# Two places for the parts of an expert tile's tokens, and a new order around the first two expert tiles

## The chip, the cores and the metric

The kernel runs on one core of one Trainium2 chip. The metric is the device time of one execution in microseconds (us); the median of three runs is given, and one further execution was profiled. A core has TensorE (PE; its weight loads are PEld), VectorE (DVE), ScalarE (ACT), GpSimd (POOL) and SyncE (SP, which here only issues DMAs). Each engine works through its own list of instructions in order, and they meet at semaphores alone: `then_inc` raises one when an instruction has finished, `wait_ge` holds its engine until it has a value.

## The reference

Three layers over 2304 tokens of width 512, all in float32:

```python
scores = q @ k.T / 8                          # 4 batches x 8 heads, 576 tokens, 64 wide
attn = softmax(scores where >= the 32nd largest of the row)
x = attn @ v                                  # 2304 x 512
x = softplus(x @ w_in) @ w_out                # 512 -> 2048 -> 512
logits = x @ w_gate                           # 8 experts
e = argmax(logits);  gate = softmax(logits)[e]
out = gate * (relu(x @ w1[e]) @ w2[e])        # 512 -> 1024 -> 512, the token's own expert
```

## The kernel before

Matmuls run at a fast rate that rounds its operands, so each operand is split in two parts, hi (the rounded value) and lo (what is left), and `product` adds three matmuls: hi by hi, hi by lo, lo by hi. ScalarE makes the hi part, VectorE or GpSimd the lo part.

**Attention and the dense layer** take the first three quarters. The 2304 tokens are 18 pieces of 128, and two pieces make a group of the dense layer. For each group `up` and `down` run over 8 units of w_in and w_out, with the attention of later groups between them. `down(g, u, part)` (L648) is half of a unit's down-projection, six matmuls of 512 columns; the last group's units are called by `last_down(u)`, which does both halves.

**Routing.** A piece that is done is turned (`turn_tokens`, L667) and its 8 logits are computed by `logits` (L678), four matmuls of 8 columns. From the logits VectorE makes the choice of expert (`choose`) and the gate (`gates`). TensorE counts how many tokens before each one went to the same expert: `count_early` for the first 16 pieces, `count_late` (L705) for the last two. From the counts VectorE works out for every token its tile of 128 and its lane in the tile, then TensorE makes tables of the tiles from them (`slots_early`, and `slots_late`, L712, 18 matmuls). `in_slots`, `slot_values` and `lane_hots` on VectorE make the operands of slots_late. The first two expert tiles belong to the expert with most tokens among the first 16 pieces and are filled from these, so their tables are there early.

**An expert tile T.** GpSimd gathers its 128 tokens into `xs` (an indirect DMA). TensorE turns them with `turn_xs(T, place)` (L722), four instructions into bank 0 of PSUM. ScalarE copies that out as `xsT_hi` (`xs_out`, L1013) and VectorE forms `xsT_lo` (`xs_low`, L1340). `e_up(T)` (L741) is 8 products, two halves (n) of 512 columns with four steps (kk) each, into banks 1 and 2. Their rectification is half on ScalarE (`e_relu_out`, L1020) and half on VectorE (`relu`, L1333); both raise `e_relu`. `turn_h(T)` (L764) turns the 1024 hidden values, 8 instructions into banks 3 and 4, `e_h_out` and `h_low` split them, and `e_down(T)` (L774) is 8 products. `y_out` scales by the gate and GpSimd scatters the rows. With one place for xsT_hi and xsT_lo, the tokens of the next tile can be copied out only when e_up of the tile before is done (`act.wait_ge(e_h_raw, T)`).

**The order** is written out by hand for each engine. `amid` names calls that are made ahead of a product inside another call: in `e_up` by (n, kk), in `e_down` by kk. Around the end of the dense layer TensorE does, in this order: turn_xs(0), last_down(6), the first half of e_up(0), last_down(7), the second half of e_up(0) with the turns and logits of the last two pieces in it, turn_xs(1), turn_h(0), e_up(1) with count_late after its first product, e_down(0) with turn_h(1) and slots_late at its products 4 and 5, e_down(1). VectorE does in this stretch: the lo parts of the first expert's weights (`first_w1`, `first_w2`), relu(0), choose, xs_low(1), gates, the chain from the counts to `abs_tile`, h_low(0), in_slots, slot_values, lane_hots, relu(1), and after slots_late the tables, h_low(1) and y_out(0). For the later tiles all engines run the same loop: on TensorE turn_h(T), e_up(T+1), turn_xs(T+2), e_down(T).

The SBUF space behind xsT_lo was an unused gap of the size of both parts.

Of the kernel before, what the change touches and what calls it, by code (L numbers as in the profile page):

```python
# [20 lines left out]
def build(nc, q, k, v, w_in, w_out, w_gate, w1, w2, out):  # L21
# [97 lines left out]
    with ExitStack() as ctx:  # L119
        def sb(name, shape, dt=F32):  # L120
            return ctx.enter_context(nc.sbuf_tensor(name, shape, dt))
# [87 lines left out]

        wbuf = sb("wbuf", [P, 3, WLEN])  # L210
        sb("gap_d", [P, WLEN])
        xsT_hi = sb("xsT_hi", [P, KD, P], F32R)
        xsT_lo = sb("xsT_lo", [P, KD, P], F32R)
        sb("gap_x", [P, 2 * KD * P])
        xs = sb("xs", [P, XS, DM])
        inslot = sb("inslot", [P, NT, 4, NTAB], F32R)
        hr = sb("hr", [P, EF])
# [329 lines left out]
        def _(pe):  # L547
# [121 lines left out]
            def turn_tokens(g, kk, bank):  # L669
                nonlocal turns  # L670
                pe.wait_ge(y_copied, kk + 1)
                if bank == 5:
                    pe.wait_ge(h_copied, UNITS * (g + 1))
                turns = kk + 1
                for m in range(KD):
                    mm = nc.tensor.transpose(psum[:, bank, m * P:(m + 1) * P],
                                             x2tok[:, kk % 2, m * P:(m + 1) * P], ident[:])
                mm.then_inc(turned, 1)  # L678

            def logits(kk, bank):  # L680
                nonlocal logit_turns
                if kk == 0:
                    pe.wait_ge(wg_loaded, 16)
                pe.wait_ge(turn_copied, kk + 1)
                for m in range(KD):
                    mm = nc.tensor.matmul(psum[:, bank, 0:E], x2T[:, kk % 2, m, :], wg[:, m, :],
                                          start=(m == 0), stop=(m == KD - 1))
                mm.then_inc(logits_raw, 1)
                logit_turns = kk + 1
# [31 lines left out]
            def turn_xs(T, place):  # L721
                pe.wait_ge(gathered[place], T // XS * 16 + 16)  # L722
                if not (isinstance(T, int) and T == 0):
                    pe.wait_ge(xs_split, T)
                for kk in range(KD):
                    mm = nc.tensor.transpose(psum[:, 0, kk * P:(kk + 1) * P],
                                             xs[:, place, kk * P:(kk + 1) * P], ident[:])
                mm.then_inc(xs_turned, 1)
# [4 lines left out]
            def product(ps, x_hi, x_lo, par, at, start, stop):  # L733

                hi = w_hi[:, par * 2, at:at + 512]
                lo = wbuf[:, par * 2, at:at + 512].bitcast(F32R)
                nc.tensor.matmul(ps, x_hi, hi, start=start, stop=False)  # L737
                nc.tensor.matmul(ps, x_hi, lo, start=False, stop=False)  # L738
                return nc.tensor.matmul(ps, x_lo, hi, start=False, stop=stop)  # L739

            def e_up(T, rank=None, amid=(), halves=False, parts=(0, 1)):  # L741
                rank = rank_at(T) if rank is None else rank
                if halves and 0 in parts:
                    pe.wait_ge(quarter_split, 2)
                elif not halves:
                    pe.wait_ge(w1_split, rank + 1)
                if 0 in parts:
                    pe.wait_ge(xs_split, T + 1)
                    if not (isinstance(T, int) and T == 0):
                        pe.wait_ge(e_relu, T * 2)  # L750
                par = rank % 2
                for n in parts:
                    if n and halves:
                        pe.wait_ge(quarter_split, 3)
                        pe.wait_ge(w1_split, 1)
                    for kk in range(KD):
                        if (n, kk) in amid:
                            amid[n, kk]()
                        mm = product(psum[:, 1 + n, :], xsT_hi[:, kk, :], xsT_lo[:, kk, :], par,
                                     kk * EF + n * 512, kk == 0, kk == KD - 1)  # L760
                if 1 in parts:
                    mm.then_inc(e_h_raw, 1)
# [60 lines left out]
            def last_down(u):  # L823
                for part in range(2):
                    down(LASTG, u, part)

            up(LASTG, 0)
            for part in range(2):
# [20 lines left out]
            rank_first = rank_at(0)  # L849
            turn_xs(0, 0)  # L850
            last_down(6)
            e_up(0, rank_first, halves=True, parts=(0,))
            last_down(7)
            e_up(0, rank_first, {(1, 1): lambda: turn_tokens(LASTG, NT - 2, 5),
                                 (1, 2): lambda: turn_tokens(LASTG, NT - 1, 4),
                                 (1, 3): lambda: logits(NT - 2, 3)}, halves=True, parts=(1,))
            logits(NT - 1, 7)
            turn_xs(1, 1)
            turn_h(0)
            e_up(1, rank_first, {(0, 1): count_late})  # L860
            e_down(0, 0, rank_first, {KE // 2: lambda: turn_h(1), KE // 2 + 1: slots_late}, halves=True)
            e_down(1, 1, rank_first, {KE - 2: lambda: turn_xs(2, 2)})
            pe.wait_ge(tiles_ready, 1)
            e_up(2)
            turn_xs(3, 3)
            _, live = live_below(pe)

            def tile(T, place, live):
                turn_h(T)
                with live(T + 1):  # L870
                    e_up(T + 1)
                with live(T + 2):
                    turn_xs(T + 2, (place + 2) % XS)
                e_down(T, place % 2)
# [5 lines left out]
        def _(act):  # L880
# [98 lines left out]
            def logits_out(kk, bank):  # L979
                act.wait_ge(logits_raw, kk + 1)  # L980
                nc.scalar.copy(lg[:, kk, :], psum[:, bank, 0:E]).then_inc(logits_copied, 1)
# [28 lines left out]
                act.wait_ge(w2_loaded[0] if n else w2_first, 32)  # L1010
                nc.scalar.copy(w_hi[:, 0, at], wbuf[:, 0, at]).then_inc(w2_hi if n else first_hi, 1)

            def xs_out(T):  # L1013
                act.wait_ge(xs_turned, T + 1)
                if not (isinstance(T, int) and T == 0):
                    act.wait_ge(e_h_raw, T)
                nc.scalar.copy(xsT_hi[:].rearrange("p k t -> p (k t)"),
                               psum[:, 0, :]).then_inc(xs_copied, 1)

            def e_relu_out(T):  # L1020
# [91 lines left out]
                first_w1((u - 3) // 2, (u - 3) % 2)  # L1112
            rectify(LASTG, 7)
            logarithm(LASTG, 7)
            xs_out(0)
            h_high(LASTG, 7)
            first_w2(0)
            first_w2(1)
            down_out(LASTG)
            turn_out(NT - 2, 5)  # L1120
            turn_out(NT - 1, 4)
            logits_out(NT - 2, 3)
            logits_out(NT - 1, 7)

            e_relu_out(0)
            xs_out(1)
            gate_exps(1)
            e_h_out(0, 0)
            e_relu_out(1)
            e_h_out(1, 1)  # L1130
            xs_out(2)
            act.wait_ge(splits_ready, 1)
            early_split(act, 1, split_w1)
            next_expert(act, 1, split_w2)
# [2 lines left out]
            def tile(T, place, live):  # L1137
                e_relu_out(T)
                with live(T + 1):
                    xs_out(T + 1)  # L1140
                e_h_out(T, place % 2)
                early_split(act, T, split_w1)
                with live(T + 1):
                    next_expert(act, T, split_w2)
# [4 lines left out]
        def _(dve):  # L1149
# [187 lines left out]
                nc.vector.tensor_scalar(hr[:, 512:EF], psum[:, 2, :], 0.0, None,  # L1337
                                        ALU.max).then_inc(e_relu, 1)

            def xs_low(T):  # L1340
                dve.wait_ge(xs_copied, T + 1)
                nc.vector.tensor_tensor(xsT_lo[:].rearrange("p k t -> p (k t)"), psum[:, 0, :],
                                        xsT_hi[:].rearrange("p k t -> p (k t)").bitcast(F32),
                                        ALU.subtract).then_inc(xs_split, 1)

            def h_low(T, hpar):
# [34 lines left out]

            for q in range(4):
                first_w1(q // 2, q % 2)
            xs_low(0)
            first_w2(0)
            first_w2(1)

            relu(0)
            dve.wait_ge(logits_copied, NT)
            choose(LAST, 1)  # L1390
            xs_low(1)
            gates(LAST, 1)
            dve.wait_ge(counts_ready, 2)
            then(nc.vector.tensor_copy(new_count[:].rearrange("p t e -> p (t e)"),
# [13 lines left out]
            then(nc.vector.tensor_reduce(abs_tile[:], pos3[:], AX.X, ALU.add))  # L1408
            then(nc.vector.tensor_tensor(abs_tile[:], abs_tile[:], reltile[:], ALU.add))
            h_low(0, 0)  # L1410
            in_slots(inslot, abs_tile, slice(0, NT), NTAB)
            slot_values(inslot, slice(0, NT), NTAB)
            lane_hots(LAST).then_inc(lanes_ready, 1)
            relu(1)

            then(nc.vector.tensor_tensor(prod[:], perm[:], bc(need[:], EE, 1), ALU.mult))
            then(nc.vector.tensor_reduce(ntile[:], prod[:], AX.X, ALU.add))
# [34 lines left out]
                then(nc.vector.tensor_tensor(prod[:], match[:], bc(values, EE, 1), ALU.mult))  # L1452
                then(nc.vector.tensor_reduce(by_rank[:, i, :], prod[:], AX.X, ALU.add))
            nc.vector.tensor_copy(by_rank_i[:], by_rank[:]).then_inc(ranks_ready, 1)
            xs_low(2)
            y_out(1, 1)


# [16 lines left out]
            early_split(dve, 1, split_w1)  # L1475
            next_expert(dve, 1, split_w2)
            relu(2)
            xs_low(3)
            _, live = live_below(dve)

            def tile(T, place, live):
                h_low(T, place % 2)
                early_split(dve, T, split_w1)
                with live(T + 1):
                    next_expert(dve, T, split_w2)
                    relu(T + 1)
                with live(T + 2):
                    xs_low(T + 2)
                y_out(T, place)

            later_tiles(dve, tile, live)
# [203 lines left out]
```

## Time and profile before

| | us |
|---|---|
| median of three runs | 1056.23 (1055.35 to 1056.42) |
| profiled execution | 1057.04 |
| its span, first to last instruction | 1054.8 |
| TensorE busy in the span | 992.9 |
| VectorE busy | 817.3 |
| ScalarE busy | 727.6 |
| GpSimd busy | 711.9 |

The span is what the trace shows; the execution's own time is 2.2 us longer. Times in a timeline count from the start of the span. A row gives start, duration, engine, line, operation, output<-inputs and the number of like instructions merged into it; in brackets stands the engine's idle time before it and what ended it. Matmuls overlap: the distance from one start to the next is what one costs, not its duration. The granted clock of TensorE (PEclk) is a share of 2.4 GHz; it has two levels here, 1.00 and 0.50, and its mean over the span is 0.983.

### The profile page before, as it was taken

The numbers are of one execution on the slowest core, as the hardware profiler recorded it, in microseconds if no ns is written. First come the engines' busy times: TensorE is split into PE (matmuls) and PEld (weight loads), VectorE is DVE, ScalarE is ACT, GpSimd is POOL, SyncE is SP. The second block draws the span as 40 slices with busy tenths as digits, with TensorE's granted clock in tenths as the row PEclk, the third lists the DMA queues.
The fourth block names the chain that finished last, engine by engine and source line by source line (L and its number), as shares of the span: only waits on it lengthen the run. The fifth ranks groups of instructions, "written<-read, shape, count | busy, mean of one in ns | idle before, by whom it ended". The sixth has DMA issues, their size and how long they took to land.

```text
span 1054.8 us, 21596 instructions
## 1 busy us (share of the span) xinstructions
PE 992.9 (94%) x6878; PEld 806.3 (76%) x6879; DVE 817.3 (77%) x1744; ACT 727.6 (69%) x1390; POOL 711.9 (67%) x831
## 2 busy tenths in 40 slices
PE   5565899999999999999999999999999999999996
PEld 2343687788788788788788888887887788888875
DVE  7999999999999999999999999994345622222261
ACT  3888898988998998998888999998554111111140
POOL 2688898889899899899888899899351311111101
PEclk9996899999999999999999999999999999999999
DMA  9723253343344343324434333333481421111100
GB/s 311 257 91 127 112 171 121 128 143 121 114 153 165 114 157 121 124 98 144 169 119 155 117 120 102 121 121 121 156 331 54 165 96 52 40 40 40 40 20 20
DMA packets 43391, 130.99 MB, mean 124 GB/s; under 512 B 4320, under 2 KB 18656, under 8 KB 33056
## 3 DMA queue, kind: packets, MB, share of 16 engines
q1 hardware_dynamic: 40256, 120.09, 32.5%
q0 software_dynamic: 3040, 9.70, 2.7%
q8 instruction: 51, 0.84, 0.3%
q14 instruction: 44, 0.36, 0.1%
HBM read 111.95 MB, written 18.09 MB: 123 GB/s over the span
## 4 chain that ended last, share of the span: by engine, by line
PE 80%; DVE 8%; POOL 4%; ACT 3%; issue 3%; DMA 1%; SPq 1%; ACTq 0%; DVEq 0%; POOLq 0%
PE psum L614 8%; PE psum L575 7%; PE psum L644 7%; PE psum L737 6%; PE psum L739 6%; PE psum L738 6%; PE psum L646 6%; PE psum L645 6%; PE psum L663 6%; PE psum L665 6%; PE psum L664 6%; PE psum L589 5%; DVE top L1158 3%; DVE work L1164 3%; PE psum L769 2%
## 5 line engine op out<-in xcount | busy, mean ns | idle before, releaser
L1158 DVE MAX8 top<-work 128x8 f32<-128x576 f32 x432 | 305.4, 752 | 0.0
L1164 DVE MATCH_REPLACE8 work<-top,work 128x576 f32<-128x576 f32 x288 | 212.6, 749 | 0.0
L644 PE MATMUL psum<-x_parts,wi_hi 128*128 128x256 f32 x576 | 171.1, 297 | 0.0
L645 PE MATMUL psum<-x_parts,wi_hi 128*128 128x256 f32 x576 | 162.9, 283 | 0.0
L646 PE MATMUL psum<-x_parts,wi_lo 128*128 128x256 f32 x576 | 162.7, 283 | 0.0
L614 PE MATMUL psum<-prT,vtok 128*64 128x128 f32 (+3 forms) x1600 | 117.1, 287 | 15.2 <-ACT prT L918 15.2
L614 PEld LDWEIGHTS psum<-prT,vtok 128*64 128x64 f32 (+1 forms) x1600 | 85.5, 144 | 54.2 <-issue 41.2
L575 PE MATMUL psum<-kT,qT 64*128 64x512 f32 (+3 forms) x640 | 113.0, 480 | 11.5 <-DMA qT<-in_q 4.4
L1638 POOL DMA_INDIRECT out<-ys,dst_now x19 | 19.2, 1012 | 152.6 <-DVE ys L1360 150.7
L663 PE MATMUL psum<-wo_ring,h_hi 128*128 x288 | 119.1, 414 | 1.0 <-POOL h_lo L1547 0.9
L1541 POOL TENSOR_TENSOR hs<-hs,ab 128x512 f32<-128x512 f32 x72 | 93.7, 1301 | 32.7 <-ACT ab L941 32.5
L644 PEld LDWEIGHTS psum<-x_parts,wi_hi 128*128 128x128 f32 x576 | 109.9, 191 | 6.8 <-issue 2.4
L905 ACT ACTIVATE pr<-pr,bias 128x576 f32<-128x576 f32 x144 | 110.0, 766 | 6.7 <-POOL pr L1536 3.7
L665 PE MATMUL psum<-wo_ring,h_lo 128*128 x288 | 113.1, 393 | 0.0
L664 PE MATMUL psum<-wo_ring,h_hi 128*128 x288 | 112.7, 391 | 0.0
L645 PEld LDWEIGHTS psum<-x_parts,wi_hi 128*128 128x128 f32 x576 | 110.1, 191 | 0.2
L646 PEld LDWEIGHTS psum<-x_parts,wi_lo 128*128 128x128 f32 x576 | 110.1, 191 | 0.0
L911 ACT ACTIVATE pr<-pr,rden 128x576 f32<-128x576 f32 x144 | 104.4, 784 | 8.0 <-DVE rden L1175 8.0
L575 PEld LDWEIGHTS psum<-kT,qT 64*128 64x128 f32 (+1 forms) x640 | 57.5, 195 | 68.1 <-issue 59.4
L589 PE MATMUL psum<-ident,pr 128*128 128x128 f32 x576 | 81.3, 284 | 22.3 <-ACT sc L890 16.7
L1547 POOL TENSOR_TENSOR h_lo<-hs,h_hi 128x512 fp32r<-128x512 f32 x72 | 93.1, 1293 | 5.9 <-ACT h_hi L949 5.9
L589 PEld LDWEIGHTS psum<-ident,pr 128*128 128x128 f32 x576 | 66.6, 145 | 27.9 <-issue 17.6
(215 smaller groups left out, 2353.1 us busy)
## 6 DMA issues: line engine op xcount, KB each, us to landing
wo_ring<-wo_parts SPq DMA_DIRECT2D x72, 1024.0 KB, 4.8
wo_parts<-wo_ring SPq DMA_DIRECT2D x8, 1024.0 KB, 3.8
kT<-in_k SPq DMA_DIRECT2D x16, 288.0 KB, 3.4
qT<-in_q SPq DMA_DIRECT2D x16, 288.0 KB, 3.9
vtok<-in_v SPq DMA_DIRECT2D x16, 256.0 KB, 2.9
wo_raw<-in_moe_w_out SPq DMA_DIRECT2D x1, 4096.0 KB, 14.1
wi_raw<-in_moe_w_in SPq DMA_DIRECT2D x4, 1024.0 KB, 14.4
x_rows<-x2tok SPq DMA_DIRECT2D x16, 256.0 KB, 2.4
```

The source lines that it names most:

```text
L575: mm = nc.tensor.matmul(to[rows, :], qT[h * HD:(h + 1) * HD, p, cols], kT[h * HD:(h + 1) * HD, p, keys], start=True, stop=True)
L589: mm = nc.tensor.transpose(transit[:, j // 3, j % 3 * P:(j % 3 + 1) * P], pr_of(n)[:, first_key(t) + c * P:first_key(t) + (c + 1) * P], id ...
L614: mm = nc.tensor.matmul(x_raw_at[h * HD:(h + 1) * HD, cols], vtok[rows, p, c, h * HD:(h + 1) * HD], probs, start=(c == 0), stop=(c == FULL))
L644: nc.tensor.matmul(ps[:, part, :], wi_hi[:, u, kk, f], hi, start=first, stop=False)
L645: nc.tensor.matmul(ps[:, part, :], wi_hi[:, u, kk, f], lo, start=False, stop=False)
L646: mm = nc.tensor.matmul(ps[:, part, :], wi_lo[:, u, kk, f], hi, start=False, stop=last)
L663: nc.tensor.matmul(psum[:, 6 + a, :], high, hi, start=(f == 0), stop=False)
L664: nc.tensor.matmul(psum[:, 6 + a, :], high, lo, start=False, stop=False)
L665: mm = nc.tensor.matmul(psum[:, 6 + a, :], low, hi, start=False, stop=(f == KF - 1))
L905: nc.scalar.activation(pr[:, n % 2 * 2 + t, :], pr[:, n % 2 * 2 + t, :], ACT.Exp, bias=bias[:, n % 2, 0, t:t + 1], scale=1.0, accum_out=ep ...
L1158: nc.vector.max(top[:, at, 8 * r:8 * r + 8], sc_of(n)[:, t, :] if r == 0 else work[:, t, :]).then_inc(topk_step, 1)
L1164: nc.vector.match_replace(work[:, t, :], top[:, at, 8 * r - 8:8 * r], sc_of(n)[:, t, :] if r == 1 else work[:, t, :], TAKEN).then_inc(topk ...
```

## The change

The two parts get a second place, chosen by the tile's number, odd or even; e_up, xs_out and xs_low take it as an argument, and xs_out now waits for e_up of two tiles before. On TensorE turn_xs(1) moves between the two halves of the last down-projection. E_up(1) no longer stands behind turn_h(0): turn_h(0) is now inside it, ahead of (0, 3), and count_late ahead of (1, 1). In e_down(0), turn_h(1) moves from product 4 to 5 and slots_late from 5 to 6. ScalarE does xs_out(1) before it copies out the last down-projection, and e_relu_out(0) before the last logits. VectorE does xs_low(1) before relu(0), and relu(1) between h_low(0) and in_slots.

```diff
-        xsT_hi = sb("xsT_hi", [P, KD, P], F32R)
-        xsT_lo = sb("xsT_lo", [P, KD, P], F32R)
-        sb("gap_x", [P, 2 * KD * P])
+        xsT_hi = sb("xsT_hi", [P, 2, KD, P], F32R)
+        xsT_lo = sb("xsT_lo", [P, 2, KD, P], F32R)
...
-            def e_up(T, rank=None, amid=(), halves=False, parts=(0, 1)):
+            def e_up(T, xpar, rank=None, amid=(), halves=False, parts=(0, 1)):
...
-                        mm = product(psum[:, 1 + n, :], xsT_hi[:, kk, :], xsT_lo[:, kk, :], par,
+                        mm = product(psum[:, 1 + n, :], xsT_hi[:, xpar, kk, :], xsT_lo[:, xpar, kk, :], par,
...
             turn_xs(0, 0)
             last_down(6)
-            e_up(0, rank_first, halves=True, parts=(0,))
-            last_down(7)
-            e_up(0, rank_first, {(1, 1): lambda: turn_tokens(LASTG, NT - 2, 5),
-                                 (1, 2): lambda: turn_tokens(LASTG, NT - 1, 4),
-                                 (1, 3): lambda: logits(NT - 2, 3)}, halves=True, parts=(1,))
+            e_up(0, 0, rank_first, halves=True, parts=(0,))
+            down(LASTG, UNITS - 1, 0)
+            turn_xs(1, 1)
+            down(LASTG, UNITS - 1, 1)
+            e_up(0, 0, rank_first, {(1, 1): lambda: turn_tokens(LASTG, NT - 2, 5),
+                                    (1, 2): lambda: turn_tokens(LASTG, NT - 1, 4),
+                                    (1, 3): lambda: logits(NT - 2, 3)}, halves=True, parts=(1,))
             logits(NT - 1, 7)
-            turn_xs(1, 1)
-            turn_h(0)
-            e_up(1, rank_first, {(0, 1): count_late})
-            e_down(0, 0, rank_first, {KE // 2: lambda: turn_h(1), KE // 2 + 1: slots_late}, halves=True)
+            e_up(1, 1, rank_first, {(0, 3): lambda: turn_h(0), (1, 1): count_late})
+            e_down(0, 0, rank_first, {KE // 2 + 1: lambda: turn_h(1), KE - 2: slots_late}, halves=True)
             e_down(1, 1, rank_first, {KE - 2: lambda: turn_xs(2, 2)})
             pe.wait_ge(tiles_ready, 1)
-            e_up(2)
+            e_up(2, 0)
             turn_xs(3, 3)
             _, live = live_below(pe)
 
             def tile(T, place, live):
                 turn_h(T)
                 with live(T + 1):
-                    e_up(T + 1)
+                    e_up(T + 1, (place + 1) % 2)
...
-            def xs_out(T):
+            def xs_out(T, xpar):
                 act.wait_ge(xs_turned, T + 1)
-                if not (isinstance(T, int) and T == 0):
-                    act.wait_ge(e_h_raw, T)
-                nc.scalar.copy(xsT_hi[:].rearrange("p k t -> p (k t)"),
+                if not (isinstance(T, int) and T < 2):
+                    act.wait_ge(e_h_raw, T - 1)
+                nc.scalar.copy(xsT_hi[:, xpar].rearrange("p k t -> p (k t)"),
...
             rectify(LASTG, 7)
             logarithm(LASTG, 7)
-            xs_out(0)
+            xs_out(0, 0)
             h_high(LASTG, 7)
             first_w2(0)
             first_w2(1)
+            xs_out(1, 1)
             down_out(LASTG)
             turn_out(NT - 2, 5)
             turn_out(NT - 1, 4)
             logits_out(NT - 2, 3)
+            e_relu_out(0)
             logits_out(NT - 1, 7)
 
-            e_relu_out(0)
-            xs_out(1)
             gate_exps(1)
             e_h_out(0, 0)
             e_relu_out(1)
             e_h_out(1, 1)
-            xs_out(2)
+            xs_out(2, 0)
...
-                    xs_out(T + 1)
+                    xs_out(T + 1, (place + 1) % 2)
...
-            def xs_low(T):
+            def xs_low(T, xpar):
                 dve.wait_ge(xs_copied, T + 1)
-                nc.vector.tensor_tensor(xsT_lo[:].rearrange("p k t -> p (k t)"), psum[:, 0, :],
-                                        xsT_hi[:].rearrange("p k t -> p (k t)").bitcast(F32),
+                nc.vector.tensor_tensor(xsT_lo[:, xpar].rearrange("p k t -> p (k t)"), psum[:, 0, :],
+                                        xsT_hi[:, xpar].rearrange("p k t -> p (k t)").bitcast(F32),
...
-            xs_low(0)
+            xs_low(0, 0)
             first_w2(0)
             first_w2(1)
 
+            xs_low(1, 1)
             relu(0)
             dve.wait_ge(logits_copied, NT)
             choose(LAST, 1)
-            xs_low(1)
             gates(LAST, 1)
...
             h_low(0, 0)
+            relu(1)
             in_slots(inslot, abs_tile, slice(0, NT), NTAB)
             slot_values(inslot, slice(0, NT), NTAB)
             lane_hots(LAST).then_inc(lanes_ready, 1)
-            relu(1)
...
-            xs_low(2)
+            xs_low(2, 0)
...
-            xs_low(3)
+            xs_low(3, 1)
...
-                    xs_low(T + 2)
+                    xs_low(T + 2, place % 2)
```

## Rows read from the trace of the kernel before

**Rows 1.** The page, part 1: busy us, share of span, instructions by engine.
```profile
PE 992.9 (94%) x6878; PEld 806.3 (76%) x6879; DVE 817.3 (77%) x1744; ACT 727.6 (69%) x1390; POOL 711.9 (67%) x831
```

**Rows 2.** Windows, later tiles: us, busy (xcount) PE, PEld, DVE, ACT, POOL, PEclk, DMA, GB/s.
```profile
960.00:1000.00 40.00, 40.00 (x193) 32.99 (x192) 10.27 (x15) 6.44 (x12) 7.24 (x12) 1.00 0.12 39
```

**Rows 3.** Timeline of TensorE: start, duration, instruction, idle before and its releaser.
```profile
806.05 0.95 PE L686 MATMUL psum<-wg,x2T 128*128 128x8 f32 x8
...
807.76 1.91 PE L769 MATMUL psum<-ident,hr 128*128 128x128 f32 x8 [0.27 <-ACT hr L1024]
809.32 0.78 PE L737 MATMUL psum<-w_hi,xsT_hi 128*128 x1
...
810.74 0.44 PE L709 MATMUL psum<-onehot,tri 128*128 128x16 f32 x2
...
816.05 0.39 PE L739 MATMUL psum<-w_hi,xsT_lo 128*128 x1
816.57 0.49 PE L737 MATMUL psum<-w_hi,hrT_hi 128*128 x1
...
820.43 1.07 PE L769 MATMUL psum<-ident,hr 128*128 128x128 f32 x8 [0.80 <-DVE hr L1337]
...
822.04 2.11 PE L716 MATMUL psum<-inslot,lanehot 128*128 128x108 f32 x18
...
826.26 0.47 PE L737 MATMUL psum<-w_hi,hrT_hi 128*128 x1
```

**Rows 4.** Timeline of VectorE, the same stretch.
```profile
798.07 4.50 DVE L1378 TENSOR_TENSOR wbuf<-wbuf,w_hi 128x2048 fp32r<-128x2048 f32 x2 [2.67 <-ACT w_hi L1011]
806.25 0.69 DVE L1337 TENSOR_SCALAR hr<-psum 128x512 f32<-128x512 f32 x1 [3.69 <-PE psum L739]
...
811.62 0.18 DVE L1394 COPY new_count<-psum 128x16 f32<-128x16 f32 x1 [1.77 <-PE psum L710]
...
815.53 1.29 DVE L1350 TENSOR_TENSOR hrT_lo<-psum,hrT_hi 128x512 fp32r<-128x512 f32 x2
...
819.16 0.42 DVE L1260 TENSOR_TENSOR lanehot<-rank,lane 128x256 fp32r<-128x256 f32 x1
819.50 0.68 DVE L1337 TENSOR_SCALAR hr<-psum 128x512 f32<-128x512 f32 x1
...
825.44 1.28 DVE L1350 TENSOR_TENSOR hrT_lo<-psum,hrT_hi 128x512 fp32r<-128x512 f32 x2
```

**Rows 5.** Timelines of ScalarE (ACT), then of GpSimd (POOL).
```profile
801.49 1.08 ACT L970 COPY x2tok<-psum 128x512 f32<-128x512 f32 x2 [1.64 <-PE psum L665]
...
807.10 0.60 ACT L1024 ACTIVATE hr<-psum 128x512 f32<-128x512 f32 x1
...
787.88 0.98 POOL L1625 DMA_INDIRECT xs<-x_rows,src_now  x1 [0.81 <-POOL src_now L1621]
...
824.64 0.18 POOL L1621 COPY src_now<-src_i 128x1 int32<-128x1 int32 x1 [27.03 <-DVE src_i L1431]
```

**Rows 6.** Windows about the clock's fall; PEclk stands before the DMA share.
```profile
804.50:807.80 3.30, 3.04 (x25) 2.67 (x23) 1.18 (x4) 0.98 (x5) 0.00 (x0) 1.00 0.00 0
807.90:811.20 3.30, 3.30 (x14) 3.01 (x14) 1.78 (x9) 1.67 (x4) 0.00 (x0) 0.50 0.02 5
811.30:830.00 18.70, 17.77 (x89) 14.19 (x89) 15.28 (x56) 1.67 (x3) 2.89 (x6) 1.00 0.08 24
```

**Rows 7.** Chain of waits in order of time: start, us, what; full clock.
```profile
756.62 0.49 PE psum L694 x2
757.11 0.22 PE psum L695 x2
...
846.36 0.44 PE psum L726 x4
...
852.18 0.23 PE psum L739
852.41 0.87 PE psum L769 x8
```

## The prediction

> **What bounds the kernel now.** The line of busy time comes first: TensorE works 94% of the span, VectorE 77% [rows 1]. The stages come next, since that share is a mean. While the later expert tiles run (960 to 1000 us) TensorE is busy 40.00 of 40 us, and every instruction that the change touches in the loop over tiles stands there: the places of an expert tile's tokens alternate, but who waits for what, in which order on each engine, stays [rows 2]. Xs_out(T+1) gets a weaker wait on ScalarE, yet e_relu_out(T) ahead of it in the same queue waits for the same matmuls. So the loop can give nothing and lose nothing, and what is won or lost before it arrives at the end in full. That leaves the passage from the last down-projection to the start of e_down(1), 800 to 827 us. There I read the engines one by one: TensorE [rows 3], VectorE [rows 4], ScalarE and GpSimd [rows 5].
>
> What the reader is to see: turn_h(0) starts at 807.76, 0.06 after ScalarE's rectification, which itself stood behind logits_out. Count_late starts at 810.74. From 811.62 VectorE is on one chain: counts, ranks, abs_tile, then h_low(0) at 815.53, and e_down(0) starts at 816.57, when its first half is done. E_up(1) had ended, at 816.3. Then in_slots, lane_hots (ending 819.58), relu(1) (819.50), which turn_h(1) waits for at 820.43 (0.80 idle), slots_late at 822.04, tables, h_low(1) at 825.44, e_down(1) at 826.26. So the passage alternates between TensorE's order and VectorE's chain, and the chain cannot begin before count_late.
>
> **The change, part by part.** Sums are made against the profiled execution: 1057.04 us, span 1054.8, 2.2 outside it. It lies 0.81 above the median of 1056.23.
>
> *Second turn of tokens moved up.* Turn_xs(1) goes ahead of the second half of down(7). It costs TensorE 0.44 warm [rows 7], nothing else: its gather was issued at 787.88, 12 us earlier, and no DMA or GpSimd instruction moves. All behind it up to the end of e_up(0) slides by 0.44: the last matmuls whose end VectorE's relu(0) waits for then end at 806.69 instead of 806.25. On ScalarE xs_out(1) (128x512, the 0.60 of the like rectification; between 801.0 and 801.6) fits into the 1.64 idle ahead of down_out, which wants 801.49 + 0.44 = 801.93. On VectorE xs_low(1), 0.69 as relu, runs at 802.6 behind first_w2, in the 3.69 idle before relu(0). Were that cover gone, down_out and all behind it would be up to 0.6 late. The stores of the last rows go 0.44 later; the gather that needs them waits for the tables until 824.64, 22 us behind. Cost 0, all in the 0.44.
>
> *E_up(1) ahead of turn_h(0).* This is what the second places allow. Relu(0) ends on VectorE at 807.38; ScalarE's, no longer behind logits_out, at 807.3. With 0.2 for the wait (0.06 from ScalarE's relu to turn_h(0), 0.35 from h_low's first half to e_down(0)) e_up(1) starts at 807.6, against 809.32.
>
> *Count_late moved from behind one product to behind five.* A product is three matmuls, 0.23 each [rows 7], 0.70 together before rounding; the first after a pause takes 0.1 more. Nine matmuls: 807.6 + 0.1 + 2.1 = 809.8. Turn_h(0): 0.87 warm [rows 7], 810.66. Two products: 812.06. Count_late 0.45 warm, estimated: 0.63 at the lower clock, and a like four with 128 columns each, where it has 16, took 0.49 + 0.22 [rows 7]. It ends at 812.5. VectorE picks up the counts at 812.65, against 811.62: **1.0 later**. At one clock it would be 2.6 later; in the execution before, TensorE's granted clock was 0.50, its lower level of 1.2 GHz, from 807.9 to 811.3 [rows 6], after sixteen logits matmuls of 8 columns, a turn and a wait of 0.27. Its turn_h took 1.56 instead of 0.87 (807.76 to 809.32), its first product 1.42 instead of 0.70, its count some 0.2 more: 1.6 in all. Now full products stand in that place at once, a turn less stands among the small matmuls and the wait is shorter; I take the clock as staying at 2.4 GHz there. If it falls, those 1.6 come back.
>
> *The xs_low(1) taken out of the chain after choose.* 0.69 off VectorE at 808.3, but VectorE is done with the gates 1.77 before the counts at 811.62; logits_out comes 0.44 later and even so the gates end near 810.1. Worth 0, since count_late is the later.
>
> *H_low(0), then relu(1), then tables.* The chain from counts to h_low(0) is unchanged, 3.91: e_down(0) starts at 816.57 + 1.0 = 817.6. E_up(1) ends at 814.7 (812.5 + nine matmuls), so TensorE waits some 2.8 where it waited 0.3. Relu(1), 0.60, now precedes in_slots: lanes are ready at 819.58 + 1.0 + 0.6 = 821.2.
>
> *Turn_h(1) one product later, slots_late one more.* From 817.6: five products 3.6, turn_h(1) 0.87 with no wait (it saves the 0.80), one product 0.70, so slots_late starts at 822.8, after the lanes. Before: 822.04. **0.75 later.** Its 1.95, the tables and h_low(1) follow as before: the first half of h_low(1), 825.44 + 0.69 before, is there at 826.13 + 0.75 = 826.9. E_down(0) has ended by 826.3, because only two products are left behind slots_late, not three. E_down(1) starts at 827.0 to 827.2, against 826.26: **0.75 to 0.95 later, I take 0.8**. The gather of tile 2, turn_xs(2), xs_low(2) and e_up(2) hang on the same tables and slide alike.
>
> *Second places in SBUF, other addresses in the loop.* No row has a price. From below and above: the later tiles take 40.00 of 40, so there is no idle to take away; a slower read would show in the matmuls' 0.23, of which I see no reason for a change. 0.
>
> Sum: 0 + 0.8 = 0.8 us, 1057.8 in the terms of the profiled execution, **1057.0** against the median.
>
> **The clock, weighed against the Trainium skill.** The row shows the fall at 807.9 and the return by 811.3 [rows 6]; idle alone didn't make it, for 0.80 idle at 819.6 was followed by full clock. The Trainium skill, "TensorE: Matmul & The Clock Gate", Part 1, says that half rate is the default and that activity lifts it, and its Part 4 that turns don't count as busy in the same way. The trace agrees with both as far as it goes. By that rule the 2.8 us of waiting that the change opens is a danger, and the rival below comes out.
>
> **Rivals.**
> 1. *The clock falls in the new wait before e_down(0).* Place: 814.7 to 817.6. The wait is ten times the 0.27 before the fall at 807.76, which speaks for it; against it, full matmuls stand on both sides, and waits of 0.8 passed unharmed. Price: one stretch like that of 807.9 to 811.3, 3.4 at half rate, costs 1.7, on a path that TensorE alone sets up to slots_late. 0.8 + 1.7 = 2.5: 1058.7. With 0.8 lost already it decides once the fall costs 1.3 more, 2.6 us at the lower level.
> 2. *The early fall stays,* inside e_up(1). 1.6 come back: 1058.6. For: logits are still there. Against: the products. Some of the timed executions of before may also have escaped their fall (their spread is 1.07), to the same effect on the difference.
> 3. *TensorE's order decides, not VectorE's chain.* If the counts reached VectorE early enough to hide the chain, TensorE alone would need from 807.6: e_up(1) with turn_h and count 7.1, e_down(0) with turn_h and slots 8.7 with its first matmul: 823.4 instead of 826.26, 2.9 faster: 1053.3. Against it stands the chain of 3.91 + 0.7 behind a count at 812.5. It wants count_late first, and the change puts it last.
>
> **How the numbers follow.** Forecast 0.62, rival 1 0.20, rival 2 0.08, rival 3 0.08, and 0.02 for nothing moved at all. A measurement of this kernel tells about 0.2%, 2.1 us, from no change. The forecast lies within; rivals 1 and 2 mostly beyond (0.23 with their part of the edges), rival 3 is faster. Same 0.68, slower 0.24, faster 0.08. The range runs from 1055.0 (the forecast less an uncertainty of 1.0 in the waits and the 1.0 spread of the runs) to 1059.2 (rivals 1 and 2 with 0.5 on top). The forecast's own range is 1055.8 to 1058.2.
>
> **What would show it.** Right: turn_xs(1) between two halves of down(7) at 0.44; e_up(1) 0.2 after the rectifications; the clock at 1.00 from 804 to 814; the counts' first VectorE instruction 1 us later; an idle of 2.5 to 3 us before e_down(0), released by hrT_lo; no idle before turn_h(1); under 1 us before e_down(1); the later tiles at 40.00 of 40. Wrong: an idle under 1.5 before e_down(0); a clock of 0.50 behind it; the loop's matmuls off 0.23; or a wait for xs_low(1).

## The result, and the profile after

| | us |
|---|---|
| changed kernel, median of nine runs | 1059.37 (1058.29 to 1060.30) |
| kernel before, median of nine runs beside them | 1056.12 (1055.35 to 1058.16) |
| ratio | 1.0030, 95% interval 1.0019 to 1.0040 |
| profiled execution of the changed kernel | 1058.81, span 1056.6 |

Slower by some 3.2 us, where 0.8 was forecast: 1059.37 against a forecast of 1057.0 and a range up to 1059.2. A second timing on another occasion gave a ratio of 1.0028 (1.0017 to 1.0038), 1058.87 against 1056.19.

The profile page's row of busy time and the window over the later tiles, which answer to [rows 1] and [rows 2], read in the changed kernel:

```profile
PE 993.5 (94%) x6878; PEld 806.7 (76%) x6879; DVE 817.3 (77%) x1744; ACT 727.8 (69%) x1390; POOL 711.9 (67%) x831
```

```profile
960.00:1000.00 40.00, 40.00 (x195) 32.99 (x194) 11.66 (x17) 7.52 (x14) 7.24 (x12) 1.00 0.13 40
```

TensorE's work is the same and the loop over the later tiles is as full as before. So the time went in the passage. TensorE there, answering to [rows 3] (start, duration, instruction, in brackets the idle time before it):

```profile
799.47 0.60 PE L725 MATMUL psum<-ident,xs 128*128 128x128 f32 x4
799.83 0.48 PE L662 MATMUL psum<-wo_ring,h_hi 128*128 x1
...
806.06 0.95 PE L685 MATMUL psum<-wg,x2T 128*128 128x8 f32 x8
807.09 0.47 PE L736 MATMUL psum<-w_hi,xsT_hi 128*128 x1
...
809.24 1.04 PE L768 MATMUL psum<-ident,hr 128*128 128x128 f32 x8
...
811.51 0.29 PE L708 MATMUL psum<-onehot,tri 128*128 128x16 f32 x2
...
813.80 0.40 PE L738 MATMUL psum<-w_hi,xsT_lo 128*128 x1
816.98 0.49 PE L736 MATMUL psum<-w_hi,hrT_hi 128*128 x1 [2.78 <-DVE hrT_lo L1349]
...
818.03 0.63 PE L736 MATMUL psum<-w_hi,hrT_hi 128*128 x1
818.45 0.63 PE L737 MATMUL psum<-wbuf,hrT_hi 128*128 x1
...
822.14 1.03 PE L768 MATMUL psum<-ident,hr 128*128 128x128 f32 x8
...
823.71 2.11 PE L715 MATMUL psum<-inslot,lanehot 128*128 128x108 f32 x18
...
827.93 0.47 PE L736 MATMUL psum<-w_hi,hrT_hi 128*128 x1 [0.65 <-DVE hrT_lo L1349]
```

Turn_xs(1) stands at 799.47, between the two halves of down(7), and costs TensorE 0.48 (forecast: 0.44): from the first matmul of down(7) to the first one behind it is 3.19, against 2.71 before. E_up(1) starts at 807.09, right behind the rectifications. The turn before (0, 3) is at full clock and count_late comes at 811.51. Then TensorE stands idle for 2.78 us, released by h_low(0), and behind that wait the matmuls start 0.42 apart, not 0.23. VectorE, answering to [rows 4], shows why e_down(0) waits: the counts are picked up at 812.13 after 2.48 us of idle, and h_low(0) follows 3.91 later, as before; relu(1) follows it at once.

```profile
812.13 0.17 DVE L1393 COPY new_count<-psum 128x16 f32<-128x16 f32 x1 [2.48 <-PE psum L709]
...
816.04 1.29 DVE L1349 TENSOR_TENSOR hrT_lo<-psum,hrT_hi 128x512 fp32r<-128x512 f32 x2
817.24 0.68 DVE L1336 TENSOR_SCALAR hr<-psum 128x512 f32<-128x512 f32 x1
```

The clock of the changed kernel, answering to [rows 6] (the value before the last two):

```profile
807.90:811.20 3.30, 3.30 (x20) 2.82 (x19) 1.23 (x8) 1.29 (x3) 0.00 (x0) 1.00 0.02 5
811.30:816.90 5.60, 2.90 (x15) 2.12 (x13) 4.26 (x19) 0.60 (x1) 0.00 (x0) 1.00 0.00 0
817.50:820.90 3.40, 3.40 (x9) 2.62 (x9) 3.33 (x8) 0.00 (x0) 0.00 (x0) 0.50 0.00 0
```

The fall among the logits is gone, and there is one behind the new wait: 9 matmuls in 3.4 us. ScalarE's copy of the last down-projection, 801.49 in [rows 5], stands at 801.50 here and serves below as the mark from which the passage is measured: over the fourteen profiles of all kernels it lies anywhere from 801.3 to 803.3, and what stands behind the start of e_up(2) took 222.0 to 222.2 in all of them.

```profile
801.50 1.08 ACT L969 COPY x2tok<-psum 128x512 f32<-128x512 f32 x2 [0.81 <-PE psum L664]
```

The first matmul of e_up(2) ends the passage, at 834.44: 32.94 from the mark. In the kernel before it is 832.78, so 31.29. Turn_xs(1) stands ahead of the mark in the changed kernel and behind it before, which adds 0.48 (from the first matmul of down(7) to the mark it is 3.39 against 2.91). These two executions thus differ by 1.65 + 0.48 = 2.13.

### The profile page after: what moved, and what is told of

Same layout as the page of the kernel before. It is cut to its first block, busy times and chain, and to the rows that moved or that the text cites. A ratio compares the mean times of both kernels' runs of the same rounds, so it can differ in the third digit from the quotient of the medians.

```text
span 1056.6 us, 21595 instructions
## 1 busy us (share of the span) xinstructions
PE 993.5 (94%) x6878; PEld 806.7 (76%) x6879; DVE 817.3 (77%) x1744; ACT 727.8 (69%) x1390; POOL 711.9 (67%) x831
## 4 chain that ended last, share of the span: by engine, by line
PE 81%; DVE 7%; POOL 4%; ACT 3%; issue 3%; DMA 1%; SPq 1%; ACTq 0%; DVEq 0%; POOLq 0%
PE psum L613 8%; PE psum L574 7%; PE psum L643 7%; PE psum L736 6%; PE psum L738 6%; PE psum L737 6%; PE psum L645 6%; PE psum L644 6%; PE psum L662 6%; PE psum L664 6%; PE psum L663 6%; PE psum L588 5%; DVE top L1157 3%; DVE work L1163 3%; PE psum L768 2%
```

## Experiments

Each kernel was timed beside the kernel before, and rows with the same value under "before" were timed together. Ratios are to it, with 95% intervals.

| kernel | median | before | ratio |
|---|---|---|---|
| early count | 1055.47 | 1056.66 | 0.9989 (0.9980 to 0.9998) |
| wait filled | 1058.30 | 1056.66 | 1.0018 (1.0009 to 1.0027) |
| relu(1) back | 1058.74 | 1056.66 | 1.0023 (1.0014 to 1.0032) |
| first half of the change | 1056.31 | 1056.66 | 0.9995 (0.9986 to 1.0004) |
| changed kernel again | 1058.87 | 1056.19 | 1.0028 (1.0017 to 1.0038) |
| early count, early slots | 1054.54 | 1056.19 | 0.9984 (0.9974 to 0.9993) |
| count one product earlier | 1058.23 | 1056.32 | 1.0019 (1.0010 to 1.0028) |
| early count and slots, relu(1) back | 1055.78 | 1056.32 | 0.9996 (0.9987 to 1.0005) |

**Early count.**

```diff
-            e_up(1, 1, rank_first, {(0, 3): lambda: turn_h(0), (1, 1): count_late})
+            e_up(1, 1, rank_first, {(0, 2): count_late, (0, 3): lambda: turn_h(0)})
```

> The changed kernel with one thing different: count_late stands ahead of (0, 2) of e_up(1), behind two products, instead of ahead of (1, 1), behind five and turn_h(0). Theory A (VectorE's chain from the counts makes the wait before e_down(0), and the lower clock follows that wait): the counts reach VectorE 3 us earlier, e_down(0) starts without a wait at 814 to 815, the clock reads 1.00 behind it, and the time is 3.5 to 5 us under the changed kernel's, so 1 to 2 under the one before. Theory B (the second places and the other addresses, or the turn inside the down-projection, cost most of the 3.2 us): under 1 us faster than the changed kernel.

It is 1.2 us under the kernel before, where the changed kernel is 2.7 to 3.2 over it: 3.9 to 4.4 between them, as expected. TensorE at e_down(0):

```profile
815.08 0.49 PE L736 MATMUL psum<-w_hi,hrT_hi 128*128 x1 [0.40 <-DVE hrT_lo L1349]
```

The wait is 0.40, not quite the none that was expected, and no fall shows in the passage. VectorE in this kernel says what bounds the counts now:

```profile
810.03 0.16 DVE L1243 TENSOR_TENSOR gate_parts<-gate,gate_parts 128x2 fp32r<-128x2 f32 x1
810.23 0.17 DVE L1393 COPY new_count<-psum 128x16 f32<-128x16 f32 x1
```

The last gate instruction runs straight into the counts, without idle: with the gates where they stand, an earlier count still would gain nothing. The counts lie 8.19 behind the mark (802.04) here and 10.63 in the changed kernel, 2.44 earlier, and the passage of 28.95 is 2.44 shorter than the changed kernel's without a fall (31.39, below): the passage follows the counts. Theory B, a cost of the second places or the moved turn, has fallen.

**The wait filled.** Ten matmuls that nothing reads, into the bank of the tokens, which is free there.

```diff
             e_up(1, 1, rank_first, {(0, 3): lambda: turn_h(0), (1, 1): count_late})
+            for x in range(10):
+                nc.tensor.matmul(psum[:, 0, :], xsT_hi[:, 1, x % KD, :],
+                                 w_hi[:, rank_first % 2 * 2, x % KD * EF:x % KD * EF + 512], start=True, stop=True)
```

> The changed kernel with ten extra matmuls of 512 columns, whose result nothing reads, between e_up(1) and e_down(0), where TensorE waits 2.8 us. They leave VectorE's chain as it is. Theory A with the clock: the wait shrinks to about 0.4 us, e_down(0) starts at the same place, the clock reads 1.00 behind it, and the time is 1.3 to 1.7 us under the changed kernel's. Rival (the wait alone costs, the clock's fall is paid for elsewhere or was chance of this one profile): no difference, within 0.4 us. Theory B: the same as the rival.

TensorE in the filled kernel:

```profile
814.00 2.43 PE L861 MATMUL psum<-w_hi,xsT_hi 128*128 x10
816.95 0.50 PE L736 MATMUL psum<-w_hi,hrT_hi 128*128 x1 [0.51 <-DVE hrT_lo L1352]
...
822.13 2.11 PE L715 MATMUL psum<-inslot,lanehot 128*128 128x108 f32 x18
```

and its clock over the place of the fall:

```profile
817.50:820.90 3.40, 3.40 (x18) 2.74 (x17) 3.33 (x8) 0.00 (x0) 0.00 (x0) 1.00 0.00 0
```

E_down(0) starts where it did (816.95 against 816.98), 18 matmuls stand where 9 stood, and slots_late starts at 822.13, 1.58 earlier than in the changed kernel, whose mark lies at the same place. In the trace it is worth what was expected. Timed it is worth less: against the kernel before it is 1.6 us slower, where the changed kernel was 3.2 and 2.7 slower in its two timings, so 1.0 to 1.6 is gained; against the kernel with relu(1) back, which was timed together with it, only 0.4, the edge of what the rival expected, and the intervals overlap. An execution that had no fall can gain nothing from the fill, and the repeated profiles below show such executions.

**Relu(1) back** behind lane_hots in the changed kernel.

```diff
             h_low(0, 0)
-            relu(1)
...
             lane_hots(LAST).then_inc(lanes_ready, 1)
+            relu(1)
```

> The changed kernel with relu(1) on VectorE back behind lane_hots. Theory A: lane_hots ends 0.6 us earlier, but slots_late stands 3 us behind it in the trace of the changed kernel, and turn_h(1) finds relu(1) done at 820.9 against its start at 822.1: no difference, within 0.4 us. Rival (relu ahead of the tables is what costs): 0.6 us faster or more.

Its passage is 32.97 (801.28 to 834.25), against 32.94: nothing, as expected. Its wait of 2.78 and the fall behind it are the changed kernel's. The timing is less clear: it is 2.1 us slower than the kernel before, 0.6 to 1.2 nearer to it than the changed kernel was in its own two timings. That is what the rival expected, but the intervals overlap, and in the trace no wait became shorter.

**The first half of the change alone.** Second places, turn_xs(1) inside the down-projection, and ScalarE's and VectorE's order up to xs_low(1); then the old order:

```diff
-            e_up(1, 1, rank_first, {(0, 3): lambda: turn_h(0), (1, 1): count_late})
-            e_down(0, 0, rank_first, {KE // 2 + 1: lambda: turn_h(1), KE - 2: slots_late}, halves=True)
+            turn_h(0)
+            e_up(1, 1, rank_first, {(0, 1): count_late})
+            e_down(0, 0, rank_first, {KE // 2: lambda: turn_h(1), KE // 2 + 1: slots_late}, halves=True)
```

(with relu(1) behind lane_hots again)

> The first half of the change alone: second places, turn_xs(1) between the halves of the down-projection, ScalarE's and VectorE's order up to xs_low(1); but turn_h(0) ahead of e_up(1), count_late behind its first product, turn_h(1), slots_late and relu(1) as in the kernel before. Theory A: the counts reach VectorE 1.5 to 2.5 us earlier than in the kernel before (no turn and no wait among the small matmuls), e_down(0) has no long wait, and the time is 1 to 2.5 us under the kernel before. Theory B: 1 us or more over the kernel before.

It is no slower than the kernel before and not measurably faster: 0.35 us, where 1 to 2.5 were expected. The expectation took the fall in the first profile for what every execution of the kernel before does. In the profile the passage is 29.33 (802.95 to 832.28), with the 0.48 of the turn 29.81: 1.5 under the first profile of the kernel before but only 0.3 under those without a fall, which came next. So the first half, the second places among it, is harmless, and the loss of the change is in its second.

**The two kernels again.** The kernel before was profiled three times more, the changed one twice.

> The kernel before, unchanged, profiled once more, to see how often its clock falls in the passage. From the start of the last down-projection's last unit (798.58 in the first profile) to the end of the span it took 256.2 us there, with the lower clock from 807.9 to 811.3. If the fall belongs to the order of the work, it is here again and the stretch takes 256.0 to 256.4; if it is chance, the stretch without it takes 254.5 to 255.0 and part of the 3.2 us of the timed runs is explained by executions of the kernel before without the fall.

> The same once more: 256.0 to 256.4 with the fall, 254.5 to 255.0 without.

> The kernel before, profiled a fourth time. Of three profiles one had the lower clock in the passage; x2tok to e_up(2) took 31.28 us with it and 30.15 and 30.13 without. Expected: one of the two.

> The changed kernel, unchanged, timed again beside the kernel before and profiled once more. By the passage alone (258.5 us in its first profile against 256.2) it is 2.2 us slower than the kernel before; by its first timing 3.2. Theory A: 2 to 3.5 us slower, and the clock falls behind the wait again (258.5) or, where it escapes, the stretch takes 256.9 to 257.1, as with the filled wait.

> The changed kernel, profiled a third time. x2tok to e_up(2) took 32.94 us with the fall behind the wait, 31.39 without. Expected: one of the two, rather with the fall.

| profile | mark to e_up(2) | lower clock in the passage |
|---|---|---|
| before, first | 31.29 | 807.9 to 811.3 |
| before, a, b, c | 30.15, 30.13, 30.11 | none |
| changed, first | 32.94 | 817.5 to 820.9 |
| changed, again | 31.39 | none |
| changed, again b | 32.94 | 819.1 to 822.5 |
| relu(1) back (same wait) | 32.97 | 817.3 to 820.7 |

The profile that the forecast was read from was the odd one of four. In the kernel before, third repeat, the same turn_h(0) behind the same 0.27 of idle runs at full clock, and the gates end 0.61 us before the counts. The 0.23 of idle ahead of e_up(1), for which the trace names no releaser, fits its wait for xs_low(1) (`xs_split` in the program): that ends at 809.03, 0.10 before the first matmul, and the same 0.10 lies there in repeats a and b.

```profile
807.81 1.09 PE L769 MATMUL psum<-ident,hr 128*128 128x128 f32 x8 [0.27 <-ACT hr L1024]
809.13 0.47 PE L737 MATMUL psum<-w_hi,xsT_hi 128*128 x1 [0.23 <-issue]
```

```profile
808.34 0.69 DVE L1342 TENSOR_TENSOR xsT_lo<-psum,xsT_hi 128x512 fp32r<-128x512 f32 x1
...
809.75 0.16 DVE L1244 TENSOR_TENSOR gate_parts<-gate,gate_parts 128x2 fp32r<-128x2 f32 x1
...
810.52 0.17 DVE L1394 COPY new_count<-psum 128x16 f32<-128x16 f32 x1 [0.61 <-PE psum L710]
```

In the changed kernel, profiled again, the clock stays up behind the same wait of 2.78 us, and the two windows about the wait, moved by the 1.8 by which its mark lies later, differ from the first profile's in that alone:

```profile
813.10:818.70 5.60, 2.91 (x15) 2.13 (x13) 4.25 (x19) 0.60 (x1) 0.00 (x0) 1.00 0.00 0
819.30:822.70 3.40, 3.40 (x17) 2.71 (x17) 3.33 (x8) 0.00 (x0) 0.00 (x0) 1.00 0.00 0
```

```profile
818.79 0.49 PE L736 MATMUL psum<-w_hi,hrT_hi 128*128 x1 [2.78 <-DVE hrT_lo L1349]
```

With no fall on either side the change costs 31.39 + 0.48 - 30.13 = 1.74. A fall costs the kernel before 1.16 and the changed one 1.55. If it comes in one of four executions before and in three of four after (the last row counted, though its kernel is not quite the same), the difference is 1.74 + 0.75 x 1.55 - 0.25 x 1.16 = 2.6, inside both timed intervals (2.0 to 4.2 and 1.8 to 4.0 us). So few profiles give the two shares only roughly: 2.6 is an estimate. Without any fall after the change it would be 1.45, which is outside both intervals.

The same sum (passage + 0.48 - 30.13 - 0.25 x 1.16), with no fall assumed in the experiment's kernel, gives for the early count -1.0 (timed -1.2), for the first half -0.6 (-0.35), for the filled wait 1.5 (1.6), and for the two kernels below with early slots -1.7 (-1.65) and -0.6 (-0.5). The sum holds where the long wait is gone or filled. For relu(1) back it gives 3.0 with the fall in every execution and 1.5 with it in none; timed, 2.1 lies between.

**Count one product earlier.**

```diff
-            e_up(1, 1, rank_first, {(0, 3): lambda: turn_h(0), (1, 1): count_late})
+            e_up(1, 1, rank_first, {(0, 3): lambda: turn_h(0), (1, 0): count_late})
```

> The changed kernel with count_late one product earlier, ahead of (1, 0). Theory A: the counts, and with them e_down(0) and all behind it, come 0.7 us earlier; the wait before e_down(0) shrinks from 2.8 to 2.1 us. From the copy of the last down-projection (x2tok) to the start of e_up(2) it takes 30.7 us if the clock does not fall behind the wait, against 31.4 for the changed kernel without the fall; 32.2 with it. The timed gain over the changed kernel is 0.7 us, or up to 2.2 where the shorter wait also keeps the clock up. Rival (the wait is set by something else than the counts): the wait stays 2.8 us.

```profile
817.55 0.50 PE L736 MATMUL psum<-w_hi,hrT_hi 128*128 x1 [2.09 <-DVE hrT_lo L1349]
```

A wait of 2.09, a passage of 30.73 (802.77 to 833.50), no fall: 0.66 under the changed kernel's 31.39. One product, 0.7, moves the whole passage nearly one to one. Timed it is 1.9 us over the kernel before, 0.8 to 1.3 nearer to it than the changed kernel. The sum above gives only 0.8 for it without a fall, below its interval (1.1 to 3.0), so the fall probably still comes in some of its executions; the one profile can't say in how many.

**Early count, early slots.** The early count, and

```diff
-            e_down(0, 0, rank_first, {KE // 2 + 1: lambda: turn_h(1), KE - 2: slots_late}, halves=True)
+            e_down(0, 0, rank_first, {KE // 2: lambda: turn_h(1), KE // 2 + 1: slots_late}, halves=True)
```

> The changed kernel with count_late ahead of (0, 2) of e_up(1), and turn_h(1) and slots_late back at products 4 and 5 of e_down(0). Theory A: with the early count the lanes are ready at 818.8 and slots_late need not stand behind six products; the 0.65 us wait before e_down(1) goes, and the time is 0.5 to 0.8 us under that of the kernel with the early count alone (1055.5), so near 1054.8. Rival (the order inside e_down(0) is worth nothing while VectorE's tables follow at once): within 0.3 us of it.

```profile
815.14 0.49 PE L736 MATMUL psum<-w_hi,hrT_hi 128*128 x1 [0.40 <-DVE hrT_lo L1349]
818.04 1.03 PE L768 MATMUL psum<-ident,hr 128*128 128x128 f32 x8
819.62 2.11 PE L715 MATMUL psum<-inslot,lanehot 128*128 128x108 f32 x18
```

The passage is 28.26 (802.09 to 830.35), 0.7 under the early count alone, as expected. Timed it is 1.65 us under the kernel before, where the early count alone was 1.2 under it; the intervals of these two overlap.

**The same with relu(1) back** behind lane_hots, by the edit shown above.

> The kernel with the early count and slots_late at product 5, with relu(1) back behind lane_hots. Theory A: now turn_h(1) is the one that comes first: e_up(1) ends at 814.7, relu(1) would end at 818.9 instead of 816.0, turn_h(1) wants it at 817.9, so TensorE waits about 1 us there and the time is 0.5 to 1.0 us over the kernel with relu(1) ahead of the tables (lane_hots gains 0.6, which slots_late can use only in part). Rival (relu's place is worth nothing, as it was behind the late count): within 0.3 us.

```profile
818.81 1.06 PE L768 MATMUL psum<-ident,hr 128*128 128x128 f32 x8 [0.90 <-DVE hr L1336]
```

The wait that the kernel before has at this turn (0.80 to 0.90 in its profiles) is back, the passage is 29.33 (801.81 to 831.14) against 28.26, and timed it is 0.5 us under the kernel before instead of 1.65: 1.1 us worse, a little more than the 0.5 to 1.0 expected. Relu ahead of the tables is worth 1.1 us behind an early count and, by the trace, nothing behind a late one.

## Why the prediction was wrong

*The steps that held.* Times of the forecast less 0.43, by which the mark came earlier than reckoned, against the trace: e_up(1) 807.17 and 807.09, count_late 811.63 and 811.51, the counts on VectorE 812.22 and 812.13, e_down(0) 817.17 and 816.98, slots_late without a fall 822.37 and 822.13 (filled wait), e_down(1) 826.67 and 826.35. The turn's 0.44 (measured: 0.48), the unchanged 3.91 of the chain, the wait of 2.8, no wait before turn_h(1), under 1 us before e_down(1), nothing in the loop: as said. The filled kernel, which is the changed one with the clock held up, is 31.41 + 0.48 - 31.29 = 0.6 over the first profile of before, for a forecast of 0.8.

*The step that failed* is the one that takes the clock out of the sum, in "Count_late moved": that the 1.6 us which the fall took in the profile were there to be saved. It failed twice. First, the fall is not a trait of the kernel before: it was in one profile of four. Without it VectorE has the counts at 810.52 (third repeat, whose mark lies 0.03 later) and not 811.62, so the change costs the passage 1.74 and not 0.8. The 0.8 was a difference to an execution that had the fall, 0.81 above the median, and it was carried over to the median as it was. The forecast noted this under rival 2, by the spread of the runs, and gave it part of 0.08. Second, the fall cost 1.16, not 1.6. The forecast counted the whole 0.69 by which turn_h(0) was slower; but at full clock e_up(1) starts at 809.13 and not at 808.7, right behind xs_low(1), which ends at 809.03 whatever the clock does (808.98 in the first profile). Of the 0.69 only about 0.2 was the fall's. (The gates end at 809.91, before the counts in both cases: they begin to bound only where the count comes early.) "At one clock" the counts come 2.1 us later in the changed kernel, both reckoned from the first matmul of down(7) (14.02 against 11.92), and not 2.6.

*Rival 1 is what the profile of the changed kernel shows,* and the sum had it at nothing: the fall behind the wait before e_down(0), priced at 1.7 and measured at 1.55 in the traces. It was given 0.20, and came in three of four profiles of that wait. It was held down by the argument that waits of 0.8 us had passed unharmed, which says nothing about one of 2.8, and by the full matmuls on both sides, which did not prevent it. Rival 1 on top of 1.74 is 3.3, the first timed difference; the forecast had it on top of 0.8.

In the Trainium skill, the rule of "TensorE: Matmul & The Clock Gate", Part 1, that idle brings half rate and activity lifts it, spoke against the change. The traces agree in the main: behind the 2.78 us wait the clock fell in three profiles of four, and with the wait filled it read 1.00. They do not prove it, since the unfilled wait read 1.00 once as well and the filled one was profiled once. The rule had deserved more than a warning. Its Part 4, on turns, no run here put to the test.

*Rival 3,* TensorE's order deciding, was right in what it named as its condition. With the count early (and slots_late early too), the chain is nearly hidden: 0.40 of wait is left before e_down(0), because the gates now bound the counts, and the kernel gains where the changed one lost. Against the first profile of the kernel before the passage is 31.29 - 28.26 - 0.48 = 2.55 shorter, of a forecast 2.9; timed the gain is 1.65, since most executions of the kernel before do not have the 1.16 of the fall to lose.

## What to carry to other kernels

Where a small operation on one engine feeds a long chain on another that ends in a wait of the first, move it by what the chain is worth, not by what fits around it: here one product less ahead of the count made the passage 0.66 us shorter, and filling TensorE earlier only made the later wait longer (2.78 us, where it had been 0.3). Before a clock's fall in a profile is entered in a sum, on either side, profile the same kernel again: the clock's level differed between executions of one kernel, and at 1.2 and 1.6 us a fall was worth nearly as much as the whole change (1.74). Price an order of instructions together with its neighbours: relu(1) ahead of the tables was worth 1.1 us or nothing, by where the count stood.

## What the runs showed of the hardware

The changed kernel, with the same 2.78 us wait at the same place, had TensorE at its lower level (granted clock 0.50, 1.2 GHz) behind it in two profiles and at 2.4 GHz in a third; the kernel with relu(1) back, with the same wait, had the lower level in its one profile. The kernel before fell in one profile of four, behind small matmuls and 0.27 us of idle that were there in all four. At the lower level matmuls of 512 columns started 0.42 us apart instead of 0.23. Executions also differed by up to 2 us ahead of the passage (the mark lay between 801.3 and 803.3 us). Nearly all of that was there by the first copy of a down-projection, at 197.8 to 199.8 us, in code that no edit touches; its cause was not looked for. It is as large as the spread of the timed runs, and it is why the passage had to be measured from a mark inside the trace.
